# Reordering the last attended chunk in the opening of a two-layer kernel: three and a half filler products out, ScalarE and VectorE pieces at other score units

## The reference

```python
for t in range(S):                                      # B=4, H=8, S=768, D=48
    cur = einsum('bhd,bhe->bhde', u * k[t], v[t])
    y[t] = einsum('bhd,bhde->bhe', r[t], state + cur)
    state = w * state + einsum('bhd,bhe->bhde', k[t], v[t])
h = x @ w_in;  x = (max(h, 0) + alpha * min(h, 0)) @ w_out
h = x @ w2_in; out = (h * tanh(softplus(h))) @ w2_out
```

## Time and profile before

| | |
|---|---|
| three runs, median | 976.9 us |
| the profiled execution | 976.2 us |
| its span, first to last instruction | 974.5 us |
| mean granted TensorE clock | 0.995 |
| TensorE busy | 965.2 us, 99% |
| VectorE, ScalarE, GpSimd busy | 68%, 64%, 38% |
| by lines of the chain that ended last | PE 97%, DVE 2%, ACT 1% |

### The profile page before, as it was taken

One profiled execution on the slowest core, in us unless ns is written; L12 is line 12 of the kernel. 1 busy time (PEld: TensorE's weight loads), 2 busy tenths in 40 slices (PEclk: granted clock), 3 DMA queues, 4 the chain that ended last, 5 costly groups with the idle time before them and its releaser, 6 DMA issues.

```text
span 974.5 us, 24246 instructions
## 1 busy us (share of the span) xinstructions
PE 965.2 (99%) x9624; PEld 789.9 (81%) x9624; DVE 661.8 (68%) x1380; ACT 623.3 (64%) x1287; POOL 370.2 (38%) x660
## 2 busy tenths in 40 slices
PE   8999999999999999999999999999999999999998
PEld 5777888888888888888888888888888888888886
DVE  7888866666666656666643437867777777677775
ACT  8766655454544555454445668878777777787775
POOL 9888886666666666666302430000000000000000
PEclk9999999999999999999999999999999999999999
DMA  4453322112211121121013330100001000000000
GB/s 132 119 184 105 104 53 89 46 47 61 80 46 46 47 78 46 48 79 33 15 40 144 98 113 33 33 33 1 33 33 34 0 32 0 24 8 0 33 1 33
DMA packets 22533, 53.25 MB, mean 55 GB/s; under 512 B 4992, under 2 KB 11040, under 8 KB 22432
## 3 DMA queue, kind: packets, MB, share of 16 engines
q1 hardware_dynamic: 20560, 42.66, 14.7%
q10 hardware_dynamic: 1872, 9.18, 2.3%
HBM read 40.12 MB, written 9.44 MB: 51 GB/s over the span
## 4 chain that ended last, share of the span: by engine, by line
PE 97%; DVE 2%; ACT 1%; issue 0%; DVEq 0%; ACTq 0%
PE acc L1152 41%; PE hid L1136 29%; PE lev L1136 10%; PE lev L1203 8%; PE tok L1226 2%; PE tok L1220 2%; PE acc L1110 1%; DVE scores L672 1%; PE tok L1177 1%; PE hid L1203 1%; PE acc L1266 0%; ACT scores L960 0%; PE acc L1351 0%; DVE power L632 0%; PE acc L1173 0%
## 5 line engine op out<-in xcount | busy, mean ns | idle before, releaser
L1136 PE MATMUL hid<-x_parts,w_hi 128*128 128x512 f32 x864 | 289.7, 390 | 0.0
L1152 PE MATMUL acc<-g_hi,w_hi 128*128 128x512 f32 x573 | 229.6, 401 | 0.0
L1152 PE MATMUL acc<-g_hi,w_lo 128*128 128x512 f32 x573 | 223.7, 390 | 0.0
L1136 PEld LDWEIGHTS hid<-x_parts,w_hi 128*128 128x128 f32 x864 | 162.2, 188 | 34.8 <-issue 0.7
L672 DVE COPY_PREDICATED scores<-mask,lev 64x128 f32<-64x128 int8 x430 | 153.5, 357 | 32.2 <-ACT scores L960 20.0
L1136 PE MATMUL hid<-x_parts,w_lo 128*128 128x512 f32 x432 | 168.2, 389 | 0.0
L1012 ACT ACTIVATE relu_neg<-hid 128x512 f32<-128x512 f32 x96 | 57.3, 596 | 163.7 <-PE hid L1136 161.7
L1152 PE MATMUL acc<-g_lo,w_hi 128*128 128x512 f32 x573 | 161.4, 390 | 0.0
L758 DVE SCALAR_TENSOR_TENSOR hid<-relu_neg,neg_slope,hid 128x512 f32<-128x512 f32 x96 | 72.5, 755 | 126.1 <-ACT hid L1013 125.7
L1152 PEld LDWEIGHTS acc<-g_hi,w_hi 128*128 128x128 f32 x573 | 107.5, 188 | 23.6 <-issue 0.2
L1152 PEld LDWEIGHTS acc<-g_lo,w_hi 128*128 128x128 f32 x573 | 107.6, 188 | 22.9
(11 more groups left out here) (125 smaller groups left out, 1363.4 us busy)
## 6 DMA issues: line engine op xcount, KB each, us to landing
w_raw<-weights SPq DMA_DIRECT2D x26, 384.0 KB, 3.5
arena<-rk_t SPq DMA_DIRECT2D x48, 192.0 KB, 3.4
arena<-rkv SPq DMA_DIRECT2D x19, 384.0 KB, 3.2
arena<-rkv SPq DMA_DIRECT2D x29, 192.0 KB, 2.6
x_dram<-result ACTq DMA_DIRECT2D x6, 768.0 KB, 3.7
arena<-x_dram SPq DMA_DIRECT2D x6, 768.0 KB, 4.4
out<-result ACTq DMA_DIRECT2D x5, 768.0 KB, 3.3
result<-weights SPq DMA_DIRECT2D x6, 384.0 KB, 3.8
```

The lines of the kernel that those rows point to most:

```text
L1136: last = nc.tensor.matmul(to[:, 0:TILE], w[:, j, kt * P:(kt + 1) * P], x[:, par, kt], start=x is x_hi and w is w_hi and kt == 0, stop=x is ...
L1152: last = nc.tensor.matmul(acc[d][:, 0:TILE], w[:, j, cols], g[:, j % RING], start=j == 0 and g is g_hi and w is w_hi, stop=j == STEPS - 1 ...
```

## The change

TensorE: fillers run only at v = 1, 3, 4, 5, 6 (out are those of v = 2, 7, 8 and the half one at the end). The last attend is split into `attend_last_known`, which zeroes the bank with two products and does all that needs neither unit 7's scores nor their padded form, and `attend_last_scores`; both stand before `sum_state(4)` instead of behind it. ScalarE: split_hi of slots 0, 1, 2 ahead of the copies of units 3, 5, 7; the clear behind the copy of unit 3; x_hi of chunk 3 ahead of `advance_state(4)`. VectorE: x_lo of chunk 3 inside the picks of unit 8, after their sixth copy; the keys of chunk 4, second half, behind those picks instead of behind unit 7's. SyncE: the loads of weight slots 3 and 4 wait for `sum_state(4)` too.

```diff
@@ -396,6 +396,7 @@
                     lo_split_reached(sp, raw_users(i)[-1])
                 elif raw_place(i) >= RAW:
                     sp.wait_ge(av_done, PER_CHUNK * CHUNKS_PER_TILE)
+                    sp.wait_ge(summed, CHUNKS_PER_TILE + 1)
                 sp.dma_start(raw_buffer(i), weights[i]).then_inc(raw_in[raw_place(i)], 16)
             def load_x2(u):
@@ -652,7 +653,7 @@
                                                           sums(tok)[:, p], ALU.mult, ALU.add)
                 last.then_inc(state_done, 2)
-            def pick_scores(v, rep):
+            def pick_scores(v, rep, between=None):
                 dve.wait_ge(score_done, v + 1)
@@ -671,6 +672,8 @@
                         done += 1
                         nc.vector.copy_predicated(dst, pick, src).then_inc(
                             pick_done if done < 2 * low_levels(rep) - 1 else mask_done, 1)
+                    if between is not None and l == 2:
+                        x_lo_part(between, 0, between, token_bank(0, between))
             def sum_diagonal(c, par):
@@ -728,12 +731,12 @@
                 dve.wait_ge(s_masks, 2 * LOW + 2)
                 for v in range(FIRST):
                     c, x = divmod(v, PER_CHUNK)
-                    pick_scores(v, 0)
-                    if 0 < v < FIRST - 1:
+                    pick_scores(v, 0, LAST if v == FIRST - 1 else None)
+                    if 0 < v < FIRST - 2:
                         keys_of(c + 1, x)
                     if x == 0 and 0 < c <= LAST:
                         x_lo_part(c - 1, 0, c - 1, token_bank(0, c - 1))
-                x_lo_part(LAST, 0, LAST, token_bank(0, LAST))
+                keys_of(CHUNKS_PER_TILE, 1)
                 sum_diagonal(by_token, by_token % 2)
             def lo_part(s, j):
@@ -976,27 +979,28 @@
             def first_tile():
-                slot_before, slot_behind = {3: 1, 7: 2}, {1: 0}
+                slots = {3: 0, 5: 1, 7: 2}
                 act.wait_ge(s_masks, 2)
                 for v in range(FIRST):
                     c, x = divmod(v, PER_CHUNK)
                     if x == 0:
                         copy_diagonal(c)
                         fill_diagonal(v)
-                    if v in slot_before:
-                        split_hi(slot_before[v])
+                    if v in slots:
+                        split_hi(slots[v])
                     copy_high(v, 0)
-                    if v in slot_behind:
-                        split_hi(slot_behind[v])
                     if v == 1:
                         act.wait_ge(s_slope, 16)
                         nc.scalar.activation(neg_slope[:], neg_slope[:], ACT.Copy, scale=-1.0).then_inc(s_negated, 1)
+                    if v == 3:
                         clear(result[:, 1:3, 0:2 * KT * HALF], zero_padded)
                     if x == 0:
                         if c < CHUNKS_PER_TILE:
                             fill_diagonal(v + 1)
+                        if c == CHUNKS_PER_TILE:
+                            x_hi_part(LAST, 0, LAST, token_bank(0, LAST))
                         advance_state(c)
-                        if c > 0:
+                        if 0 < c < CHUNKS_PER_TILE:
                             x_hi_part(c - 1, 0, c - 1, token_bank(0, c - 1))
                         if c == LAST:
                             pad_last()
@@ -1227,35 +1231,53 @@
                                                 start=begins, stop=True)
                 last.then_inc(av_done, 1)
-            def attend_last():
-
-
-
-                c, bank = LAST, token_bank(0, LAST)
-                first = c * PER_CHUNK
+            def last_places(k):
+
+                bank, span = token_bank(0, LAST), slice(CHUNK * k, CHUNK * (k + 1))
+                return ([bank[HALF * q:HALF * (q + 1), span] for q in range(2)],
+                        [bank[HALF * q:HALF * q + D, span] for q in range(2)])
+
+            def attend_last_known():
+
+                c, first = LAST, LAST * PER_CHUNK
                 pe.wait_ge(v_in[c % 2], 16 * (c // 2 + 1))
                 pe.wait_ge(state_done, 2 * (c + 1))
                 pe.wait_ge(rstate_done, first)
                 pe.wait_ge(padded_in, 2)
-                pe.wait_ge(mask_done, 2 * (first + PER_CHUNK))
+                pe.wait_ge(mask_done, 2 * (first + 1))
+                for q in range(2):
+                    nc.tensor.matmul(token_bank(0, LAST)[HALF * q:HALF * (q + 1), 0:KT * CHUNK],
+                                     zero[:].broadcast_to([P, HALF]), spread(ident[:], 1, KT), start=True, stop=False)
                 for k in range(KT):
                     x, a = divmod(k, 2)
-                    span = slice(CHUNK * k, CHUNK * (k + 1))
-                    whole = [bank[HALF * q:HALF * (q + 1), span] for q in range(2)]
-                    heads = [bank[HALF * q:HALF * q + D, span] for q in range(2)]
+                    whole, heads = last_places(k)
                     for q in range(2):
-                        nc.tensor.matmul(whole[q], v_padded[:, q, k], scores[:, (first + 1) % HELD, q, 1],
-                                         start=True, stop=False)
-                    for q in range(2):
-                        h = 2 * k + q
-                        nc.tensor.matmul(heads[q], rkv_tok[:, c % 2, 2, D * h:D * (h + 1)], scores[:, (first + x) % HELD, q, a],
+                        nc.tensor.matmul(whole[q], state_padded[0:ROWS, k], r_state[0:ROWS, 1, q, 1],
                                          start=False, stop=False)
                     for q in range(2):
                         nc.tensor.matmul(heads[q], state[0:ROWS, c % HELD, k], r_state[0:ROWS, x, q, a],
                                          start=False, stop=False)
+                    if x == 0:
+                        for q in range(2):
+                            h = 2 * k + q
+                            nc.tensor.matmul(heads[q], rkv_tok[:, c % 2, 2, D * h:D * (h + 1)],
+                                             scores[:, first % HELD, q, a], start=False, stop=False)
+
+            def attend_last_scores():
+
+                c, first = LAST, LAST * PER_CHUNK
+                pe.wait_ge(mask_done, 2 * (first + PER_CHUNK))
+                for k in range(KT):
+                    x, a = divmod(k, 2)
+                    whole, heads = last_places(k)
+                    if x == 1:
+                        for q in range(2):
+                            h = 2 * k + q
+                            nc.tensor.matmul(heads[q], rkv_tok[:, c % 2, 2, D * h:D * (h + 1)],
+                                             scores[:, (first + 1) % HELD, q, a], start=False, stop=False)
                     for q in range(2):
-                        last = nc.tensor.matmul(whole[q], state_padded[0:ROWS, k], r_state[0:ROWS, 1, q, 1],
-                                                start=False, stop=True)
+                        last = nc.tensor.matmul(whole[q], v_padded[:, q, k], scores[:, (first + 1) % HELD, q, 1],
+                                                start=False, stop=k == KT - 1)
                 last.then_inc(av_done, PER_CHUNK)
             def diagonal(c):
@@ -1269,6 +1291,7 @@
             def first_tile():
+                filled = (1, 3, 4, 5, 6)
                 pe.wait_ge(u_in, 16)
                 diagonal(0)
                 pe.wait_ge(zero_act, 1)
@@ -1278,17 +1301,18 @@
                         pe.wait_ge(s_diag, 1)
                         warm(acc[2], PAIRS // 2)
                         pe.wait_ge(zero_act, 3)
+                    if v == FIRST - 1:
+                        attend_last_known()
+                        attend_last_scores()
                     if v % PER_CHUNK == 0:
                         sum_state(v // PER_CHUNK, 0)
-                    if v > 0:
+                    if v in filled:
                         pe.wait_ge(s_diag, v // PER_CHUNK + 1)
                         warm(acc[2])
                     if v % PER_CHUNK:
                         diagonal(v // PER_CHUNK + 1)
                     if 0 < v <= LAST * PER_CHUNK:
                         attend(v - 1, 0)
-                attend_last()
-                warm(hid[1], PAIRS // 2)
             def tile1(t):
                 for j in range(STEPS):
```

## The result

Six runs of the changed kernel: median 983.92 us (983.66 to 985.42); of the kernel before, six (the three of the front among them): 976.77 us. The ratio is 1.0063 (95% interval 1.0045 to 1.008). The forecast was 974.1 us with a range up to 977.6: wrong, and by the sign. The profiled execution has a span of 982.0 us (before 974.5) and a mean granted clock of 0.985 (0.995).

A forecast was written before the change was run, and what follows sets the result against it. TensorE, busy for 99% of the span, was taken as the bound. Terms 1.8 + 1.05 + 0.63 - 0.66 = 2.82 us off the start of `up(0)`, against the 976.9 us median, gave 974.1 us; range 973.2 to 977.6.

The forecast's parts named there:

- Unit 2: Opening, unit 2: its 2.01 us filler goes, the clock still rises at 27 us, and TensorE leads by 1.65 us.
- "below zero" bound: Lower bound on the gain from unit 2's filler: below zero if the clock rises later for want of it.
- rival (b): From 27 us: clock stays low without unit 2's filler; 978.7 us for one chunk, about 981 until score(8); chance 0.12.
- Rival (a): Ahead of score(8): the clock falls again at the new wait; 976.4 us, or 975.5 if sooner back; chance 0.22.
- the wait of 0.9 us: Ahead of score(8): TensorE waits for VectorE's keys, turning 0.9 of its 2.7 us lead into a wait.
- The zeroing: Last attend: two added zeroing products, taken at 0.66 us, with an upper bound of 1.58.
- The moves that were put at nothing: Opening: reordered ScalarE splits and clear, VectorE's moved work and SyncE's later loads, covered by waits or leads; no cost.
- The saving at the last attend: From score(8) to `up(0)`: 7.62 us becomes 6.60, so 1.0 us more is gained.
- rival (c): Behind `up(0)`: thin margins and VectorE on the chain swallow 1 to 2 us of the gain; 975.5 us; chance 0.16.
- margins near zero: Behind `up(0)`: of attend(8), score(9) and GpSimd's keys, nobody is late, but two margins are near zero.

The follow-up runs named there:

- 2: The kernel before with only unit 2's filler taken out; 981.88 us, ratio 1.0037.
- 3: The changed kernel with the load of weight slot 1 moved behind the load of chunk 2's v; 983.8 us.
- 6: The changed kernel with all loads from chunk 2 on held until score(2) is done; 983.61 us, ratio 1.0033.
- 8: The changed kernel with ten two-column products put in behind unit 1's filler; 986.63 us, ratio 1.0072.
- 11: The changed kernel again, nothing changed; 984.42 us, ratio 1.0069; its profiled run took 979.52 us.
- 1: The changed kernel with unit 2's filler put back; 978.13 us, ratio 1.0012.
- 4: The kernel before with only ScalarE's new places for the three weight splits and the clear; 978.58 us, ratio 1.0003.
- 5: The kernel before with all loads from chunk 2 on held until score(2) is done; 979.4 us, ratio 1.0008.
- 7: The changed kernel with the fillers of units 2 and 7 put back; 976.99 us, ratio 0.9974.
- 10: The kernel before with only unit 7's filler taken out; 980.79 us, ratio 1.0027.
- 13: The kernel before, old order, without unit 8's filler and the half one behind the last attend; 978.4 us, ratio 1.0002.
- 12: The changed kernel with the fillers of units 2 and 7 put back, timed again with more rounds; 978.27 us, ratio 0.9992.
- 9: The changed kernel with two fillers at unit 3 instead of one; 981.9 us, ratio 1.0036.

## Why the prediction was wrong

**The step that failed** is in *Unit 2*: "The clock should still rise at 27 us". The prediction had the filler's 2.01 us as removable work because it took the clock's return for given. Without the filler the clock came back at 41.5 us. Of the profiles without a filler at unit 2, five (the changed kernel, 2, 3, 6, 8) show the clock low for 20 us, the one with two fillers at unit 3 for 10, and one (11) had come out of its first low stretch only at 22.7 us and did not fall again before 53.6. Of those with it, seven (before, 1, 4, 5, 7, 10, 13) show 7 us and one (12) 10. Adding it to the changed kernel gave 5.8 us, removing it from the old kernel cost 0.37% (0.12 to 0.62). Removing unit 7's filler cost 0.27% (0.16 to 0.37). Together that is 0.64%, and the whole change cost 0.63%. Within these intervals the two fillers account for the loss, and the rest of the change for nothing that can be told from none. The "below zero" bound was named and given too little weight, and rival (b) got 0.12.

**Rival (b)** was right in mechanism and too cheap. It priced a low-rate score 0.4 us above a full one, from the 2.15 and 2.18 us of the earlier trace rows. But those two units straddled the clock's change and were low for only part of their length. A wholly low one takes 3.13, 1.38 more. It also had no term for the diagonal products (0.71). By the chain after, the low work between 24.69 and 41.84 us costs against the same work before: two scores 0.98 and 1.38, two fillers 0.94 and 0.95, diagonal 0.71, state sums 0.81 (36.33 to 38.21, against 1.07), attends 0.85 and 0.6: 7.2 us.

**Rival (a)** was right too: the wait of 0.9 us came out as 0.77, and the clock fell behind it. It made score(8) 1.27 us longer (1.75 to 3.02), the zeroing 0.68 (0.80 to 1.48) and the known part, 59.35 to 62.42, 1.3 longer than eight pairs of 0.22: 3.3 us. The prediction's own terms for it (0.4, 0.66, 1.8 to 2.0) add up to 2.9 to 3.1, yet it entered 2.3, and put its chance at 0.22. A second fall, between 51 and 57 us, is in all eight profiles without unit 7's filler (the changed kernel, 1, 3, 6, 8, 9, 10, 11) and in none of the seven with it. The chances treated the rivals as excluding each other; both came together.

**The account.** `up(0)` is 8.69 us later after score(2)'s start than before (64.22 - 17.82 = 46.40 against 56.67 - 18.96 = 37.71; the changed execution began score(2) 1.14 us sooner). In it: stall 1.77, score(2) itself 0.2, low clock 7.2, diagonal before the wait 0.2, wait 0.77, score(8) 1.27, zeroing 1.48, the last attend's products and the state sums behind them 0.7; less the fillers, 4.74, and less 0.18 for the attend of unit 1, which was shorter than before. Sum 8.67. The stall is no cost of the change: it is also in the profiles of the kernel before with one edit (2, 4, 10 and 13). Without it 6.9 us remain, near the 7.15 by which the medians differ.

**The zeroing** was put at 0.66 us. At the full clock it measured 0.80 (kernel 12, chain), at the low 1.48. So of the two bounds, 0.66 and 1.58, the lower was the nearer; that the zeroing ran at the low rate was foreseen only in rival (a).

**The moves that were put at nothing**: ScalarE's order cost nothing that can be told from none (1.0003). VectorE's and SyncE's were not run alone.

**The saving at the last attend** (forecast 1.0 us) shows in the profile where it was sought, and is gone behind it, as **rival (c)** has it. Two profiles with a stall and one low stretch of 7 us can be compared from the stall's end to `up(0)`: kernel 4, with all fillers and the old order, 23.48 to 59.45, 35.97 us; kernel 7 21.93 to 57.04, 35.11. That is 0.86 us saved, some 0.1 of it because the low clock lasted 0.25 us less behind the stall (23.48 to 29.5 against 21.93 to 27.7). Then 1.2 us more go behind `up(0)`, in waits for GpSimd and for VectorE's picks; in kernel 12, the same kernel, it is 0.7 (977.6 - 59.05 = 918.5). The prediction had margins near zero there. That the new order makes these waits is not shown: the longest, at 79.85, stands also in kernel 5, in the old order, with 0.89 us at 79.54. By time the saving can't be told from none: 0.9974 in one job, 0.9992 in the next.

**The baseline.** The one profile of before was free of a stall that eleven of the other profiles have, and its 0.58 us of idleness made the fall look like a matter of that wait. Kernel 8 shows a fall without such a wait. The Trainium skill (TensorE: Matmul & The Clock Gate, "HAM oscillation") puts the low rate down to waits between bursts; the direction agrees for the second fall behind the wait of 0.77 us. But from 21.11 us on the chain of the changed kernel has no gap until the clock returns at 41.5, so it was not idleness that kept it low. The measurement decides. What the products of that stretch lacked is open; the runs show only that one filler more, at unit 2, shortened it.

**Open:** what decides when the q8 block is fetched, and so whether score(2) stalls. The Trainium skill (Runtime: NRT & Kernel Launch, "Instruction fetch mechanics") says that an engine's instructions come in blocks, the next being fetched while the current one runs, at a cost mostly hidden; here TensorE stood for 1.77 to 3.42 us where a q8 block came only at 18 to 21 us, and not at all where it came at 15 to 17. The link rests on their coming together in fourteen profiles; no run switched it on its own. Open too is what sets the length of the first low stretch, which by the products' durations ended before 10.3 us in fourteen profiles and at 22.7 in kernel 11.

## What to carry to other kernels

A filler product is not spare work to be counted at its duration: before taking one out, look at what the granted clock does around it, and count the rows after it at the low rate as well. Take low-rate prices only from instructions that lie wholly in the low stretch. Hold the granted clock against the durations of the products beside it, above all at the start of the span. Where an engine's lead is cut off by another engine's due time, removing a filler buys a wait, and here the wait and the fall behind it cost more than the filler (2.4 us against 1.05, kernel 10).

## What the hardware showed beyond the forecast

Score products of 48x64 slow down by 1.79 (1.75 to 3.13 us) at half the clock, and the two-column diagonal products, 0.79 us before, took 1.50 at the low rate. TensorE stood still in the same place, behind the 84th record of score(2), for 1.77 to 3.42 us, with no engine to wait for, in kernels with and without the change. And single runs of one kernel differ by up to 10 us (973.5 to 983.3 of the kernel before) with mean clocks from 0.993 to 1.000. The profiles put such differences into the opening: behind `up(0)` all fifteen lie between 917.8 and 919.1 us.
